# Four plan numbers read at a block's head, gathers issued before scatters, and the second expert weights' first loads placed around the first gather

## The reference, cut to what matters

```
attn:  y[t] = r[t] @ (state + (u*k[t]) v[t]^T);  state = w*state + k[t] v[t]^T     4 x 8 x 768 x 48
mlp:   z = leaky(y @ w_in) @ w_out              3072 x 384, 384 x 2048, 2048 x 384
moe:   compute = z @ w_skip > 0;  e = argmax(z @ w_gate);  g = softmax(z @ w_gate)[e]
       out = z;  out[compute] = z + g * (relu(z @ w1[e]) @ w2[e])      8 experts, 384 x 1024 x 384
```

## Time and profile before

| what | us |
|---|---|
| median of 3 runs | 723.09 (722.57 to 974.65) |
| the profiled execution | 722.68 |
| its span, first to last instruction | 720.9 |
| TensorE busy in it | 686.5 (95%) |
| start of the first block's transposed rows (L800) | 557.22 |
| start of the last scatter (L1720) | 713.29 |

### The profile page before, as it was taken

How to read it: one execution, slowest core, us unless ns; L and a number is a source line. 1 busy time by engine, 2 the same in 40 slices (tenths; PEclk the granted TensorE clock), 3 DMA queues, 4 the chain that set the end, 5 groups by cost and what they waited for, 6 DMA issues and landing times.

```text
span 720.9 us, 14151 instructions
## 1 busy us (share of the span) xinstructions
PE 686.5 (95%) x4359; PEld 649.5 (90%) x4360; DVE 410.8 (57%) x855; ACT 307.0 (43%) x665; POOL 101.7 (14%) x117
## 2 busy tenths in 40 slices
PE   8999999999999999999999999999996999998973
PEld 8989999999999999999999999999993789987873
DVE  8775656655656465555657555533557553745651
ACT  4455435444334433343444345333442453646630
POOL 6330000100010000001000100100101153344321
PEclk9899999999999999999999999999999899999997
DMA  8735624210422320242213222006007853383200
GB/s 243 234 113 197 197 67 132 67 50 26 129 61 67 118 78 16 59 128 67 67 48 104 55 61 87 12 15 237 12 1 252 295 202 131 113 289 136 101 20 8
DMA packets 38585, 77.43 MB, mean 107 GB/s; under 512 B 8472, under 2 KB 26806, under 8 KB 38528
## 3 DMA queue, kind: packets, MB, share of 16 engines
q1 hardware_dynamic: 33632, 62.37, 27.7%
q10 hardware_dynamic: 2432, 9.76, 3.7%
q0 software_dynamic: 2464, 4.58, 1.9%
HBM read 61.09 MB, written 12.41 MB: 102 GB/s over the span
## 4 chain that ended last, share of the span: by engine, by line
PE 85%; DVE 4%; issue 3%; ACT 3%; ACTq 2%; DVEq 1%; DMA 1%; POOL 0%; POOLq 0%
PE bank L703 29%; PE bank L721 27%; PE bank L853 6%; PE bank L807 6%; PE bank L585 4%; PE bank L641 3%; PE bank L636 3%; PE bank L654 2%; PE bank L679 1%; PE bank L834 1%; ACT w_hi L1070 1%; PE bank L592 1%; PE bank L623 1%; DMA zg<-z_rows,id_get 1%; DVE eht_lo L1570 1%
## 5 line engine op out<-in xcount | busy, mean ns | idle before, releaser
L948 ACT ACTIVATE h_sb<-bank 128x384 f32<-128x384 f32 x128 | 62.9, 492 | 250.7 <-PE bank L703 242.3
L1234 DVE TENSOR_TENSOR h_sb<-h_sb,bank 128x384 f32<-128x384 f32 x128 | 70.9, 554 | 170.4 <-ACT h_sb L948 166.7
L703 PE MATMUL bank<-x_hi,win_hi 128*128 128x384 f32 x384 | 135.5, 353 | 1.1 <-DVE win_lo L1256 1.0
L721 PE MATMUL bank<-wout_hi,g_hi 128*128 128x394 f32 x384 | 132.1, 344 | 0.0
L721 PE MATMUL bank<-wout_lo,g_hi 128*128 128x394 f32 x384 | 131.7, 343 | 0.0
L721 PE MATMUL bank<-wout_hi,g_lo 128*128 128x394 f32 x384 | 131.6, 343 | 0.0
L703 PE MATMUL bank<-x_hi,win_lo 128*128 128x384 f32 x384 | 130.5, 340 | 0.0
L703 PE MATMUL bank<-x_lo,win_hi 128*128 128x384 f32 x384 | 130.1, 339 | 0.0
L1241 DVE TENSOR_TENSOR g_lo<-h_sb,g_hi 128x384 fp32r<-128x384 f32 x128 | 71.9, 562 | 33.1 <-ACT g_hi L955 32.1
L955 ACT ACTIVATE g_hi<-h_sb 128x384 fp32r<-128x384 f32 x128 | 66.6, 521 | 41.7 <-DVE h_sb L1234 39.3
L1640 POOL DMA_INDIRECT id_list<-idgate,dst x21 | 21.3, 1014 | 446.3 <-DVE dst L1339 442.0
(11 more groups left out here) (208 smaller groups left out, 996.4 us busy)
## 6 DMA issues: line engine op xcount, KB each, us to landing
raw<-in_experts SPq DMA_DIRECT2D x32, 768.0 KB
rkt<-in_rk_t SPq DMA_DIRECT2D x46, 192.0 KB
rkn<-in_rk_nat SPq DMA_DIRECT2D x21, 384.0 KB
v<-in_v_nat SPq DMA_DIRECT2D x24, 192.0 KB, 3.0
z_rows<-z_sb SPq DMA_DIRECT2D x24, 192.0 KB, 2.7
out<-z_sb SPq DMA_DIRECT2D x24, 192.0 KB, 2.8
stage<-in_win ACTq DMA_DIRECT2D x4, 768.0 KB, 4.4
stage<-in_wout_t ACTq DMA_DIRECT2D x4, 768.0 KB, 6.4
```

The costliest lines, as they stand in the source:

```text
L703: mm = pe.matmul(h_ps[t % 2][:, 0:GT], a[:, kk, cols], b[G % 2][:, kk, :], start=n == 0, stop=n == 3 * KT - 1)
L721: mm = pe.matmul(z_ps[i][:, 0:ZW], a[t % 3][:, tok], b[:, f, :], start=f == 0 and j == 0, stop=f == FT - 1 and j == 2)
L948: act.activation(h_sb[t % 2][:], h_ps[t % 2][:, 0:GT], ACT.Copy, scale=SLOPE).then_inc(s_h_scaled, 1)
L1234: dve.tensor_tensor(h_sb[t % 2][:], h_sb[t % 2][:], h_ps[t % 2][:, 0:GT], ALU.max).then_inc(s_leaky, 1)
```

## The change

Four edits:

1. SP issues `load_w2(0)` ahead of the last group's stores, and `load_w2(1)` behind them and behind a new wait for the first gather. The later wait for two gathers becomes one for the second.
2. TensorE runs 6 idle products where 5 were.
3. TensorE reads EXPERT and PARITY of block j (now L831, L832) at the head of the block, behind those of block j+1, and no longer ahead of the second product.
4. POOL issues the gather of block j+4 ahead of the scatter of block j.

The programs of ACT and DVE, and with them the order of the splits, are the same as before.

```diff
-            store_z(GROUPS - 1)
             sp.wait_ge(s_h_done, STEPS)
             load_w2(0)
+            store_z(GROUPS - 1)
+            sp.wait_ge(rows_in[0], 16)
             load_w2(1)
...
                 if e == 2:
-                    for u in range(2):
-                        sp.wait_ge(rows_in[u], 16)
+                    sp.wait_ge(rows_in[1], 16)
...
-            idle(5)
+            idle(6)
...
                             nxt_odd = pe.value_load(plan[0:1, bass.ds(PARITY + j + 1, 1)], min_val=0,
                                                     max_val=1)
+                            cur = pe.value_load(plan[0:1, bass.ds(EXPERT + j, 1)], min_val=0, max_val=E - 1)
+                            odd = pe.value_load(plan[0:1, bass.ds(PARITY + j, 1)], min_val=0, max_val=1)
 
                             pe.wait_ge(s_relu_done, j + 1)
...
-                            cur = pe.value_load(plan[0:1, bass.ds(EXPERT + j, 1)], min_val=0, max_val=E - 1)
-                            odd = pe.value_load(plan[0:1, bass.ds(PARITY + j, 1)], min_val=0, max_val=1)
                             pe.wait_ge(s_eht_lo, 2 * j + 2)
...
                             pool.wait_ge(s_res_done, j + 1)
                             pool.sem_inc(s_pool_past, 1)
+                            with pool.If(j < blocks - UNROLL):
+                                gather(u, j + UNROLL)
                             spot_j = pool.value_load(plan[0:1, bass.ds(SPOT + j, 1)], min_val=0, max_val=SPOTS - 1)
...
-                            with pool.If(j < blocks - UNROLL):
-                                gather(u, j + UNROLL)
```

## The result

The changed kernel takes 732.26 us (median of 22 runs; the fastest 726.08) against 724.94 us for the kernel before, in runs beside it. Some executions of either kernel run longer at a lower granted clock, and the comparison leaves them out: its ratio is 1.0068, with 1.0037 to 1.0098 as 95% interval, which is 4.9 us slower, between 2.7 and 7.1. The forecast of 725.7 us stood on a base of 722.7, so it said +3.0 us; the difference lies in the interval, the time does not lie in the range of 720.0 to 728.5 us. "The same within 2%" came true.

The account below looks back on a forecast made before the run. TensorE was taken as the bound, 85% of the chain. Its terms, 1.85 - 0.3 + 1.3 + 0.2 - 0.1 = +2.95, say +3.0 us, on the profiled 722.68 us gave 725.7 us; range 720 to 728.5 us.

Parts of the forecast that it names:

- The mechanism of the heads: From second product to next transposes: four reads end after 4.4 us, transposes are due at 4.27; steady gap 0.15 us.
- Rival A: TensorE's queue is deeper than it looks, so reads at heads hide: 720.2 us, or 717.6 if the clock holds; chance 0.14.
- Blocks 1 to 5: 1.85: Heads of blocks 2, 3, 4 and 5 make TensorE 1.85 us slower; the head of 6 lies inside a wait.
- rival C: Reads themselves slow down as four meet other engines' reads, 1.5 us each instead of 0.75: 739 us; chance 0.02.
- I count -0.3 us for the whole stretch: Blocks 6 to 11: heads cost 1.85 us, moved reads and earlier rows gain 2.55, later waits limit it; net -0.3 us.
- 1.3 for the head of 12: From block 11 to 12, after a wait and a loop turn together, the transposes come 1.3 us late.
- The head of 11: Block 11's transposes come 0.95 us late after a wait, but its second product then starts about when ACT and DVE allow.
- Head of 10 and block 10's `eht_lo`: Head of 10 costs 0.15 us; block 10's second product must wait for `eht_lo`, starting at about 673.5 us.
- Gathers: POOL's gathers go about 2.1 us earlier, ending late rows in blocks 8 and 9 (0.5 us); later scatters cost nothing.
- The seam, -0.1: Ahead of the first turned rows: the gather lands earlier, but the plan's total holds them; gain 0 to 0.2, taken as 0.1.
- The clock falls again, 0: Block 0's first product stays at half clock despite the sixth idle product: gain 0, total 725.7 us; chance 0.45.
- The end, +0.2: The last scatter now has the branch ahead of it, with its register work and jump: +0.2 us.

Follow-up runs that it names:

- three_reads: Changed kernel with the EXPERT read put back ahead of the second product, PARITY left at the head: 722.71 us against 725.24 for the kernel before, ratio 0.9973.
- six_reads: Changed kernel with two more reads at each head whose values nothing uses: 744.98 us against 726.63 for the kernel before, ratio 1.0275.
- no_reads: Changed kernel with the EXPERT and PARITY reads back ahead of the second product: 722.30 us against 726.63 for the kernel before, ratio 0.9961.
- between_only: Kernel before with only its EXPERT and PARITY reads moved ahead of the wait for gathered rows: 722.83 us against 725.24, ratio 0.9969.
- filled_old_loads: Changed kernel with reads behind the first product, 8 idle products, five unused products in the last block, w2 loads in old order: 719.87 us, ratio 0.9898.
- gathers_only: Kernel before with only the gathers issued ahead of the scatters: 722.01 us against 725.24, ratio 0.9969.
- idle8: Changed kernel with EXPERT and PARITY read behind the first product, and 8 idle products instead of 6: 724.93 us against 726.39 for the kernel before, ratio 0.9970.
- reads_only: Kernel before with only the EXPERT and PARITY reads moved to the block's head: 731.38 us against 726.63, ratio 1.0046.

## Why the prediction was right or wrong

- **The mechanism of the heads: right.** Four reads are too many and three are not (`three_reads`, `six_reads`); the added waits stand where they were put, and go with edit 3 (`no_reads`). Where nothing else came in, sizes were right: 0.14, 1.00 (block 2) and 0.92 (block 7, against 4.27), foretold 0.15, 0.95, 0.95. Rival A, reads that hide, needed a queue as deep as the Trainium skill's page "TensorE: Matmul & The Clock Gate" gives in its section "Architectural detail: the array is 16× 32×32, not 1× 128×128", 64 places. The traces do not agree: the first read of a steady head never starts sooner than 1.48 us after the second product, in any of the 13 kernels (1.41 at block 13, the last).
- **The sum by stretches, "Blocks 1 to 5: 1.85": wrong in size.** It is 2.99 us. The heads of 2 to 5 measure 1.00 + 0.67 + 0.96 + 0.14 = 2.77, foretold 0.95 + 0.15 + 0.6 + 0.15. The extra is at 3 and 4: 0.52 is the read of 0.82 us in the fence above, at the head of 3; at 4 one of 0.48 us is 0.18. The prediction priced every read at the 0.75 us of one steady head, though the earlier trace rows showed reads of 0.44 and 0.56 us, and the same trace has 0.63, 1.05 and 0.98 us at 595.4, 634.4 and 674.9, at the heads of 3, 7 and 11; it met them only in rival C as a mean over all. Such reads are few, but each of them now falls on the path in full, where two reads, over 1.2 us before the transposes were due, had cover for it. Over blocks 3, 4, 9 and 12 they come to about 1.2 us. The head of 6 is no gift either: 0.12 of the 2.99.
- **"I count -0.3 us for the whole stretch", and 1.3 for the head of 12: wrong.** Foretold +1.0, measured 63.65 - 61.56 = +2.09. The gain was as foretold (2.55; the runs gave 2.3). The heads were not. Three things: (1) the head of 8, foretold 0.6, cost 1.37: its first read came at 651.5, 2.7 us after the product at 648.83 and not the 2.0 of the earlier trace rows. The wait for `eht_lo` ahead of that product ended late: the sequencer was past it at 648.6, 0.2 us ahead of the product, where it had been 1.1 ahead before (640.8, 641.92), and so the hand-over lagged. What made `eht_lo` late stands in front of it on DVE. DVE and POOL timelines, the pieces of `w_lo` ahead of block 7's `eht_lo`; first the kernel before, then the changed one.
```profile
636.23 2.36 DVE L1599 TENSOR_TENSOR w_lo<-raw,w_hi  x2 [2.97 <-ACT w_hi L1070]
637.70 3.15 POOL L1709 TENSOR_TENSOR w_lo<-raw,w_hi  x1 [1.73 <-ACT w_hi L1070]
```
```profile
642.26 4.55 DVE L1599 TENSOR_TENSOR w_lo<-raw,w_hi  x2 [2.97 <-ACT w_hi L1070]
643.25 2.48 POOL L1709 TENSOR_TENSOR w_lo<-raw,w_hi  x1 [1.26 <-ACT w_hi L1070]
```
DVE's two pieces took 2.19 us longer. Before, its second one started at 637.37, 0.33 us ahead of POOL's; in the changed kernel it started at 643.41, 0.16 us behind, and took 3.41 us instead of 1.22. TensorE's transposes, 0.92 late, can't account for that, since these pieces do not wait for them. The kernels with two or three reads at a head sort by this alone: the first read at head 8 starts 2.00 to 2.04 us after the product in the three where DVE's piece starts first (the kernel before, `between_only`, `filled_old_loads`, there by 0.04 us), and 2.69 to 2.74 us after it in the six where POOL's does. The prediction has no term for it. (2) The head of 11 was said to vanish in a wait of block 11's second product. That wait did vanish: the product at 690.95 in the fence above has none, where the earlier trace rows had 1.68. But the head cost 0.85, and second product 10 to 11 takes 10.48 us against 9.53 in `no_reads`, so TensorE and not ACT set the pace by then. (3) The head of 12 cost 1.64 for 1.3, again with one read of 0.57.
- **Head of 10 and block 10's `eht_lo`: right.** PE timeline of the changed kernel: the product waits, as said.
```profile
680.47 0.44 PE L853 MATMUL bank<-w_hi,eht_hi 128*128 x1 [0.78 <-DVE eht_lo L1570]
```
- **Gathers: right in size and place.** The later scatters cost nothing that the changed kernel shows; without edit 3 the same edit brings a wait for POOL's `w2_lo` of 1.1 to 1.5 us, of which the prediction had nothing. And the prediction added two gains, 1.25 for the reads and 0.5 for the rows, without saying that edit 4 alone gets nearly all: `gathers_only` has 2.2 of the 2.3.
- **The seam, -0.1: right, 0** in 13 traces. The plan's total and its read are what the turned rows wait for. The first gather's "3 to 4 us" was right too (3.57 at most), and, as said, did not matter.
- **The clock falls again, 0: right.** The likelier case took place, with +0.4 us of its own spread. `idle8` shows the other side: with 0.63 us of standstill it holds and the first product is 2.4 us shorter than before.
- **The end, +0.2: wrong, 0.** The tail takes 10.42 us, before 10.46. What covers the branch was not looked into.
- **Forecast and median.** Between 725.7 and 732.26 lie 6.6 us. 2.2 are the base, whose median rose from the 722.7 of the profiled execution to 724.94 in 22 runs; 1.9 are the effect, +4.9 by the ratio for +3.0; the remaining 2.4 are the difference of the two medians of all runs (7.3) over the 4.9, and 7.3 lies 0.2 outside the interval. So three steps failed: a base taken from one execution and a median of three, the price of the heads in both stretches, and a range that ended 2.8 us over the forecast, on a kernel whose runs spread over 720 to 740 us.

## What to carry to other kernels

Before putting a register read behind a product, take the time from that product's start to the sequencer's first free moment, from the trace, and count the reads that still fit; the first that does not fit costs what sticks out (0.14 us here) and every further one its whole length (0.64), in every block, and the slow ones among them are no longer averaged but paid. Look for a place with a backlog on both sides (here between the first product and the wait for rows), and if a delay has two causes in a row, try one cure alone before the two. Look, too, at pieces of work on DVE and POOL that may meet: which of them starts first by a tenth of a us decided here over 2.2 us of DVE's time. Where an engine stands still for a wait that can't be shortened, unused work in it may be worth more than moving instructions: here, in two places, it shortened two products by 3.8 us by the traces, of which 0.6 was given back in a later wait.

## What the runs showed of the hardware

- A read of the plan by TensorE's sequencer takes 0.30 us, and reads in a row start 0.75 us apart, or 0.64 where the address is not worked out anew. From the first turned rows on, 94 of 3,116 reads of all engines in the 13 traces took over 0.4 us. Of the 1,300 that met no DMA packet in flight it was one, of the others 5%. That goes together with traffic; that traffic is the cause was not tried, and remains open.
- The slow reads are more and longer where the scatter leads the gather: 13 to 16 of 232, up to 1.12 us, in the three kernels without edit 4 (`before`, `reads_only`, `between_only`), against 2 to 8, up to 0.82, in the ten with it. `gathers_only`, which differs from the kernel before by that edit alone, has 5, up to 0.57. One trace each; why was not looked into.
- A piece of `w_lo` on DVE (1.22 us alone) and one on POOL (2.34 to 2.41 us alone) do not run side by side. In all 64 cases in 13 traces where DVE's piece started while POOL's was under way, it ended 1.08 to 1.09 us after POOL's, however early it had started.
- The first gather landed in 3.58 to 3.88 us where the w2 loads stood around it (five traces), and in 5.07 to 5.43 us where both had just been issued ahead of it (five traces).
- After a standstill of 2.35 us and more the granted clock was 0.5 over the first product or a good part of it, which then took 5.95 to 7.12 us; after 0.63 us it was 1.00, and the product took 4.34 to 4.37. The last second product took 5.84 to 7.02 us behind a standstill of 4.0 to 5.6 us, and 4.43 to 4.45 behind one of 1.25.
- The clock in the first 100 us was 0.80 to 0.98 by execution, in code that all 13 kernels share, and goes along with the start of the seam, from 534.25 us (0.98) to 551.27 us (0.80). Windows of `no_reads`, same columns as above:
```profile
11.50:45.60 34.10, 34.10 (x172) 33.39 (x171) 14.54 (x24) 12.83 (x39) 7.95 (x9) 0.50 0.58 183
```
TensorE was busy all through these 34 us and still had half the clock. That is why stretches behind the seam are compared here and not spans. What starts such a stretch was not tried.
